# Another order of fills and loads at the head, a router table set in order once, and weight tiles copied two ahead

## The reference

```python
# 1. a recurrence over 768 steps, for 4 batches x 8 heads, head size 40
for t in range(S):
    y[:, :, t] = einsum('bhd,bhde->bhe', r_t, state)
    Sa    = einsum('bhde,bhe->bhd', state, a_t)
    state = state * w_t[:, :, None, :] - einsum('bhd,bhe->bhde', Sa, b_t) + einsum('bhd,bhe->bhde', v_t, k_t)
x = y as 3072 tokens of 320
# 2. first layer of experts: 8 experts, 320 -> 1024 -> 320
e_idx  = argmax(x @ w_gate);  gate = softmax(x @ w_gate)[e_idx];  eom = sigmoid(x @ w_output_gate)[e_idx]
out[token] = gate * eom * (relu(x[token] @ w1[e_idx]) @ w2[e_idx])
# 3. second layer, other weights, router w_gate2, with a capacity per expert (tokens past it give 0)
e_idx  = argmax(out @ w_gate2);  gate = softmax(out @ w_gate2)[e_idx]
out2[token] = gate * (relu(out[token] @ w1b[e_idx]) @ w2b[e_idx])
```

## Time and profile before

| | |
|---|---|
| median of 3 runs | 1327.27 us |
| the profiled execution | 1329.89 us, of which the span of the profile is 1328.1 us |
| busy in the span | PE 1088.1 us (82%), PEld 923.8, DVE 630.0 (47%), ACT 403.6 (30%), POOL 397.4 (30%) |
| granted TensorE clock, mean | 0.907 of full speed |
| chain that ended last | PE 51%, DVE 20%, DMA 11%, POOL 7%, issue 5%, ACT 3% |
| its largest lines | PE L1198 17%, PE L1179 10%, DMA of the first layer's gathers 8%, DVE L1477 6%, POOL L581 4%, DVE L1481 3% |
| L1477, 31 times | 149.4 us, 4820 ns each |
| L1481, 31 times | 87.4 us, 2820 ns each |
| stages by the timeline | head and first sets to 84 us, recurrence to 549 us, routing to 570 us, first layer to 974 us, routing to 1002 us, second layer to the end |

### The profile page before, as it was taken

How to read it: one execution, slowest core, us unless ns; L and a number is a source line. 1 busy time by engine, 2 the same in 40 slices (tenths; PEclk the granted TensorE clock), 3 DMA queues, 4 the chain that set the end, 5 groups by cost and what they waited for, 6 DMA issues and landing times.

```text
span 1328.1 us, 38352 instructions
## 1 busy us (share of the span) xinstructions
PE 1088.1 (82%) x16812; PEld 923.8 (70%) x16812; DVE 630.0 (47%) x864; ACT 403.6 (30%) x550; POOL 397.4 (30%) x278
## 2 busy tenths in 40 slices
PE   1288878787898899788688787879838999996997
PEld 0277778687788788577577676667617888875885
DVE  7546356654556451527657766757772111110111
ACT  0134333343433443133223222222103333323330
POOL 5543344423544300013332422432221121211111
PEclk9579889998988998889889988989968999998999
DMA  3433324434434221601233033212021322443000
GB/s 79 101 88 99 95 72 107 105 86 98 105 78 112 74 68 41 219 17 39 85 104 100 22 104 96 80 56 90 10 83 30 109 67 78 147 151 109 20 11 1
DMA packets 140870, 107.44 MB, mean 81 GB/s; under 512 B 89320, under 2 KB 118000, under 8 KB 140580
## 3 DMA queue, kind: packets, MB, share of 16 engines
q1 hardware_dynamic: 130560, 84.99, 23.6%
q0 software_dynamic: 6016, 16.05, 3.8%
q10 hardware_dynamic: 4132, 3.96, 1.0%
HBM read 87.51 MB, written 22.09 MB: 83 GB/s over the span
## 4 chain that ended last, share of the span: by engine, by line
PE 51%; DVE 20%; DMA 11%; POOL 7%; issue 5%; ACT 3%; SPq 1%; ACTq 0%; POOLq 0%; DVEq 0%
PE pair L1198 17%; PE pair L1179 10%; DMA y_T<-x_dram,token_all 8%; DVE AG L1477 6%; POOL AG L581 4%; DVE S_nat L1481 3%; DVE products L1265 3%; DVE T_rows L1270 3%; PE pair L1005 3%; PE pair L1186 3%; POOL abk_own L588 2%; PE pair L1166 2%; PE pair L926 2%; PE pair L1092 2%; PE pair L943 2%
## 5 line engine op out<-in xcount | busy, mean ns | idle before, releaser
L1198 PE MATMUL pair<-abk_own,H_nat 128*128 x992 | 302.6, 462 | 3.0 <-DVE S_nat L1470 1.7
L1198 PEld LDWEIGHTS pair<-abk_own,H_nat 128*128 128x128 f32 x992 | 197.2, 204 | 87.5 <-issue 25.0
L1179 PEld LDWEIGHTS pair<-H_nat,rvm 128*128 128x128 f32 x1984 | 239.8, 198 | 24.6 <-ACT H_nat L682 15.8
L1179 PE MATMUL pair<-H_nat,rvm 128*128 128x128 f32 x1984 | 241.2, 282 | 13.5 <-ACT H_nat L682 13.5
L682 ACT ACTIVATE rvm<-ring_own 128x2560 f32 x62 | 145.0, 2339 | 132.8 <-issue 80.6
L1477 DVE TENSOR_TENSOR AG<-AG,S_nat 128x2560 f32<-128x2560 f32 x31 | 149.4, 4820 | 1.1
L1470 DVE TENSOR_SCALAR S_nat<-pair,gate_all 128x320 f32<-128x320 f32 x62 | 34.2, 551 | 237.7 <-PE pair L1198 237.7
L833 ACT ACTIVATE H_nat<-pair 128x512 f32<-128x512 f32 x62 | 37.0, 597 | 329.0 <-PE pair L1186 329.0
L1463 DVE TENSOR_SCALAR H_nat<-pair 128x512 f32<-128x512 f32 x62 | 42.6, 687 | 170.3 <-PE pair L1186 170.3
L663 POOL DMA_INDIRECT between<-S_nat,token_all x31 | 35.8, 1155 | 267.1 <-DVE S_nat L1481 259.0
L581 POOL TENSOR_TENSOR AG<-abk_own,F_run 40x512 f32<-40x512 f32 x48 | 62.5, 1302 | 168.6 <-DVE T_nat L1273 152.9
(11 more groups left out here) (139 smaller groups left out, 1546.9 us busy)
## 6 DMA issues: line engine op xcount, KB each, us to landing
abk_own<-w SPq DMA_DIRECT2D x16, 1280.0 KB, 9.0
ring_own<-w SPq DMA_DIRECT2D x16, 512.0 KB, 3.5
ring_own<-w SPq DMA_DIRECT2D x32, 256.0 KB, 4.5
t_dram<-T_rows SPq DMA_DIRECT2D x12, 384.0 KB, 2.5
ring_own<-w SPq DMA_DIRECT2D x32, 128.0 KB, 5.2
w_in<-wT SPq DMA_DIRECT2D x48, 80.0 KB
abk_own<-aT SPq DMA_DIRECT2D x24, 160.0 KB
abk_own<-bT SPq DMA_DIRECT2D x24, 160.0 KB
```

The lines of the kernel that those rows point to most:

```text
L1179: mm(to, w1_now[:, par, k * F + m * P:k * F + m * P + P], xT[:, (0, 2 - m // 4)[k], :], start=(m % 4 == 0 and k == 0), stop=False, skip_gr ...
L1198: last = mm(bank[5][:, 0:DM], hidT[par][:, k, :], ring2[:, bass.ds(place, 1), k, :].rearrange("p a d -> p (a d)"), start=(k == 0), stop=(k ...
```

## The change

CLEARS falls from 6 to 4 and two fills get semaphores of their own (`abk_cleared`, `ag_cleared`): SP loads the first `a`, `b`, `k` when abk_own is clear, POOL starts when AG is clear. DVE fills AG first, makes the decays of set 0, and fills rvm, ZV and T_rows behind them (`clear_rest`). POOL's wait for the solve is left out for set 0. WARM is 9. The second router's weights are loaded to `wr_rows` as [320][8], and ACT copies them once to `wr_next` as [8][320]; L1477's product then reads both inputs with neighbouring elements. DVE waits for that copy before its first `relu1` of the first layer. `stage_w1` of the tile loop works on tile i+2 instead of i+3, in both layers; of the three copies ahead of the loop the third is dropped, and in the first layer the router copy stands in its place.

```diff
--- before.py
+++ after.py
@@ -65,7 +65,7 @@
 TABLES_IN = 16 * 2
 STEP_EXP, STEP_ONEHOT, STEP_SIG = 2, 6, 8
 AHEAD = 3
-WARM = 11
+WARM = 9
 BLK = 16
 NBLK = C // BLK
 SOLVE_STEPS = 2 * (BLK - 1) + 1
@@ -242,7 +242,8 @@
         ring2 = part(abk_own, 0, 2, FC, DM)
         A_flat = AG[:, :, :, :, :, :].rearrange("p u o b a t -> p (u o b a t)")
         terms = part(A_flat, 0, E, DM)
-        wr_next = part(A_flat, E * DM, DM, E)
+        wr_next = part(A_flat, E * DM, E, DM)
+        wr_rows = part(A_flat, 0, DM, E)
         w1_now = part(rvm[:, :, :, :, :].rearrange("p n b a t -> p (n b a t)"), 0, 2, W1_COLS)
 
         onehot, scratch, expo = (part(G_flat, n * NG * E, NG, E) for n in range(3))
@@ -269,6 +270,8 @@
 
         tables_in = sem("tables_in")
         cleared = sem("cleared")
+        abk_cleared = sem("abk_cleared")
+        ag_cleared = sem("ag_cleared")
         w_cleared = sem("w_cleared")
         ones_set = sem("ones_set")
         w_landed_in = sem("w_landed_in")
@@ -336,6 +339,7 @@
         lg_landed = sem("lg_landed")
         w_landed = sem("w_landed")
         wr_landed = sem("wr_landed")
+        wr_set = sem("wr_set")
         wr_turned = sem("wr_turned")
         router_in = sem("router_in")
 
@@ -389,7 +393,7 @@
         def fruns(k):
             return F_run[:, k % 4, :].rearrange("p (n t) -> p n t", t=C + 1)
 
-        CLEARS = 6
+        CLEARS = 4
         SLOTS = range(-3, NK + 1)
 
 
@@ -492,8 +496,10 @@
                         sp.wait_ge(f_scanned, load_set)
                     load_w(load_set)
                     if load_set == 0:
+                        sp.wait_ge(abk_cleared, 1)
+                if solves:
+                    if solve_set == 0:
                         sp.wait_ge(cleared, CLEARS)
-                if solves:
                     for u in (2 * solve_set, 2 * solve_set + 1):
                         if u >= 4:
                             sp.wait_ge(st_ready, states_upto(u - 4))
@@ -542,7 +548,7 @@
             sp.wait_ge(y_ready, NU)
             load_expert(0, 1)
             sp.wait_ge(wr_turned, 16)
-            sp.dma_start(wr_next, wr_dram.unsqueeze(0).to_broadcast([P, DM, E])).then_inc(wr_landed, 16)
+            sp.dma_start(wr_rows, wr_dram.unsqueeze(0).to_broadcast([P, DM, E])).then_inc(wr_landed, 16)
 
             for q in range(2, 2 * E):
                 s, e = divmod(q, E)
@@ -565,11 +571,12 @@
 
         @block.gpsimd
         def _(pool):
-            for t in (abk_own, T_T, S_nat):
+            nc.gpsimd.memset(abk_own[:, :], 0.0).then_inc(abk_cleared, 1)
+            for t in (T_T, S_nat):
                 nc.gpsimd.memset(t[:, :], 0.0).then_inc(cleared, 1)
             nc.gpsimd.memset(Z_diag, 0.0).then_inc(z_cleared, 1)
             nc.gpsimd.memset(D_nat[:, :], 0.0).then_inc(d_cleared, 1)
-            pool.wait_ge(cleared, CLEARS)
+            pool.wait_ge(ag_cleared, 1)
 
             def heads(t):
                 return t.rearrange("p b a t -> p (b a) t")
@@ -616,7 +623,7 @@
                 if grams:
                     pool.wait_ge(f_scanned, gram_set + 1)
                     pool.wait_ge(a_landed, 32 * (gram_set + 1))
-                    if nats:
+                    if nats and nat_set:
                         pool.wait_ge(solve_step, SOLVE_STEPS * (nat_set + 1))
                     for u in (2 * gram_set, 2 * gram_set + 1):
                         if u >= 5:
@@ -848,14 +855,15 @@
                 stage_w1(1, 1)
                 relu0(0, 0)
                 x_turned(1)
-                stage_w1(2, 0)
+                if s == 0:
+                    act.wait_ge(wr_landed, 16)
+                    copy(wr_next, wr_rows.rearrange("p d e -> p e d"), wr_set)
                 for i in range(MT):
                     if i + 1 < MT:
                         relu0(i + 1, (i + 1) % 2)
                     if i + 2 < MT:
                         x_turned(i + 2)
-                    if i + 3 < MT:
-                        stage_w1(i + 3, (i + 3) % 2)
+                        stage_w1(i + 2, i % 2)
 
 
         @block.tensor
@@ -1224,15 +1232,18 @@
             v.memset(w_in[:, ::C + 1], 0.0).then_inc(w_cleared, 1)
             dve.wait_ge(ones_set, 1)
             v.memset(ones_at[:, ::C + 1], 1.0).then_inc(ones_set, 1)
-            for t in (rvm, ZV, AG):
-                v.memset(t[:, :], 0.0).then_inc(cleared, 1)
-            v.memset(T_rows[:, :, :, :], 0.0).then_inc(rows_set, 1)
-            dve.wait_ge(tables_in, TABLES_IN)
-            dve.wait_ge(rows_set, 1)
-            v.tensor_copy(T_rows[:, :, :, BLK:2 * BLK], solve_init.unsqueeze(1).to_broadcast([P, 2, BLK, BLK])
-                          ).then_inc(rows_set, 1)
-            dve.wait_ge(cleared, CLEARS)
+            v.memset(AG[:, :], 0.0).then_inc(ag_cleared, 1)
             dve.wait_ge(ones_set, 3)
+
+            def clear_rest():
+                for t in (rvm, ZV):
+                    v.memset(t[:, :], 0.0).then_inc(cleared, 1)
+                v.memset(T_rows[:, :, :, :], 0.0).then_inc(rows_set, 1)
+                dve.wait_ge(tables_in, TABLES_IN)
+                dve.wait_ge(rows_set, 1)
+                v.tensor_copy(T_rows[:, :, :, BLK:2 * BLK], solve_init.unsqueeze(1).to_broadcast([P, 2, BLK, BLK])
+                              ).then_inc(rows_set, 1)
+                dve.wait_ge(cleared, CLEARS)
 
             def decays(k):
                 dve.wait_ge(w_landed_in, 64 * (k + 1))
@@ -1337,6 +1348,8 @@
                     m_out(2 * j)
                 if loads:
                     decays(j + 3)
+                if j == SLOTS[0]:
+                    clear_rest()
                 if chain:
                     y_out(2 * j)
                 if 0 < j <= NK:
@@ -1474,14 +1487,14 @@
                     dve.wait_ge(L["o_copied"][s], i + 1)
                     if i:
                         dve.wait_ge(lg_made, i)
-                    v.tensor_tensor(terms, wr_next.rearrange("p d e -> p e d"),
+                    v.tensor_tensor(terms, wr_next,
                                     y_rows[i % 2][:, 0:DM].unsqueeze(1).to_broadcast([P, E, DM]), ALU.mult
                                     ).then_inc(terms_made, 1)
                     dve.wait_ge(terms_made, i + 1)
                     v.tensor_reduce(y_rows[i % 2][:, DM:ROW], terms, AX_X, ALU.add).then_inc(lg_made, 1)
 
                 if s == 0:
-                    dve.wait_ge(wr_landed, 16)
+                    dve.wait_ge(wr_set, 1)
                 relu1(0, 0)
                 for i in range(MT):
                     if i + 1 < MT:
```

## The result

The changed kernel took 1225.56 us (median of 4 runs, 1220.02 to 1239.97); the kernel before, over its 4 runs, 1331.68 us. The profiled execution took 1228.57 us, its span 1226.8 us.

What follows compares the result with a forecast made beforehand. The first layer was taken as bound by a loop through DVE, POOL and DMA, not PE. From 1329.9 us profiled, -90 - 1.6 - 1.5 - 8.5 = -101.6 gave 1228 us; range 1216 to 1266.

Steps and rivals of the forecast that it cites:

- The product: DVE's L1477 in the first layer, reading neighbouring elements, falls from 4.82 us to 2.85.
- What follows from it: First layer: gather moves ahead of the next product, PE stops waiting, tiles come every 9.45 us; -93 us, net -90.
- The debit of 3 us: First layer: gathers beside experts' weight loads land later than the slack allows, 0.4 us for each of 7 loads.
- The first rival: First layer: gather stays behind the product, 14 pairs gain only 34 to 56 us, total 1262 to 1284; 28 in 100.
- The other two: Rivals: product gets no faster, 1318 us, 5 in 100; staging delays each tile's first `up`, up to 1355, 3 in 100.
- The page on POOL: Cited rule: POOL's SBUF interfaces are shared with DVE and contended by DVE instructions with two SBUF inputs, as the product remains.
- Staging two ahead: w1 copies in both layers: 0 generally, 0.8 us saved twice at second-layer experts of two tiles, -1.6 us.
- The router copy: ACT's copy ahead of the first layer's loop: 2.34 to 4.3 us long, covered before `down(0)`, cost 0.
- WARM 9: Fewer warming matmuls ahead of the routings: -1.5 us ahead of the first layer, 0 ahead of the second.
- The head: Kernel start, up to the first join: earlier first grams and POOL's wait left out, together -8.5 us.
- its two terms, -3.2 and -5.6: Head: first grams at 29.0 instead of 32.22, -3.2 us; first join no longer waiting for set 1's work, -5.6.
- my least value of 4.5: Head: smallest gain allowed for leaving out POOL's wait, since POOL now runs beside the first solve; 5.6 us was expected.

Runs made afterwards that it cites:

- the delays: Changed kernel with POOL filling a scratch buffer between the logits and each first-layer send: once, 1232.93 us; three times, 1282.23 us.
- the order alone: Kernel before, product still slow, with gather(i+4) issued ahead of send(i) instead of behind it: 1235.19 us, ratio 0.9307.

## Why the prediction was right, and where it was off

**The product** is right: 2.825 us against 2.85 taken. **What follows from it** is right, and it is the step that carried the result: D every 9.45, gathers at D - 1.0, `send` with the last one starting 311.0 us after the first gather, 92.5 less than before. Had only the product's length counted, 2 us in each of 31 tiles, the gain would have been some 60 us at most. The flip from behind to ahead of the next product is shown by the delays (3.5 us lost when the gather came 0.55 us later but still first, 53.5 when it came 2.6 later and behind the product's start) and by the order alone (89.7 us of the first layer without a faster product). The debit of 3 us for gathers beside weight loads did not fall due in the changed kernel: no later gather kept PE waiting.

**The first rival** (the gather stays behind the product) named the right mechanism and sized it from 34 to 56 us of gain; built on purpose, it left 403.5 - 364.5 = 39 us of gain in the first layer. The other two fell: the product did get faster, and no `up` of tiles 2 to 28 of the first layer waits for the copy.

**The page on POOL** (GPSIMD Engine Reference of the Trainium skill, the table of its section on specifications) was right to warn: the product with neighbouring reads, still one with two SBUF inputs, holds POOL, 3.41 instead of 1.0 where they meet.

**Staging two ahead** is right in kind. The copy ends 0.6 ahead of the end of `down`. At the experts of two tiles the next `up` starts when the copy ends:

```profile
1087.61 2.44 SPq L483 DMA_DIRECT2D ring_own<-w  x5
...
1098.77 2.34 ACT L689 ACTIVATE rvm<-ring_own 128x2560 f32 x1 [5.50 <-DMA abk_own<-w]
...
1101.21 5.18 PE L1187 MATMUL pair<-H_nat,rvm 128*128 128x128 f32 x32 [4.18 <-issue]
```

Before, a relu and an x copy stood between the earlier trace rows. The mean second layer over ten profiles with the new staging is 323.2 us, over four with the old 325.2: -2.0 against -1.6. Single profiles scatter by 2 us either way, since the `up` behind the wait ran at anything from 5.2 to 6.6 us.

**The router copy** is off in size and right in effect. ACT took

```profile
L689 ACT ACTIVATE rvm<-ring_own 128x2560 f32 x62 | 145.0, 2339 | 105.2 <-issue 85.5 <-DMA abk_own<-w 10.8 <-DMA ring_own<-w 8.9
...
L689 ACT ACTIVATE AG<-AG 128x2560 f32<-128x2560 f32 x1 | 4.9, 4860 | 0.0
```

4.86 us, 0.56 above my upper bound: ACT pays 0.98 ns for each element read 8 apart, where DVE paid 0.76. DVE's first relu waited for it until 579.14, 0.2 ahead of the end of the second `up`, and the first `down` started about 0.5 us later behind that `up` than before. So the cover was all but long enough, for a price that I had bounded from a DVE row.

**WARM 9** is the step that was wrong. I had costed it as work removed from the path, -1.5 and 0. Measured in this execution it is +1.3 and +3.9: 6.7 us off. What the step left out is what those matmuls are for. With 9 of them PE stood idle 0.8 and 2.2 us ahead of the lists' matmuls, and these then ran mostly at the lower of the two levels (1.2 instead of 2.4 GHz), 8.1 and 9.5 us, where the earlier trace rows were followed by 5.3. The first routing's lists in two stretches, with PE's busy time and behind it the granted clock:

```profile
551.83:554.50 2.67, 2.67 (x24) 1.00 0.00 0
554.50:559.91 5.41, 5.39 (x26) 0.50 0.00 0
```

The idle time is not the same in every execution. In the first routing the lists' matmuls are ready 9.8 us after the first warming matmul, in all six profiles with WARM 9. The nine warming matmuls take 8.8 to 10.0 us, the longer the later the higher clock is granted to them. So PE stood idle 0.8 to 2.4 us ahead of the eight lists that took 8.1 us or more, and not at all, 0.1, 0.7 and 1.1 ahead of the four that took 5.4 to 5.6. With WARM 11 it was at most 0.7, and all fourteen lists took 5.3 to 5.6. Idle times of 0.8 to 1.1 thus came before both. The two short lists of the profile with POOL's wait put back, after idle times of 0.1 and 1.1:

```profile
559.50 5.58 PE bank L1163 x48
...
898.10 5.58 PE bank L1163 x48
```

**The head** is right in sum (-8.4 in the mean of the profiles, -7.9 here, against -8.5; its two terms, -3.2 and -5.6, make -8.8) and was wrong in its split. After:

```profile
5.46 4.33 DVE L1235 MEMSET AG<- 128x5120 f32 x1 [1.00 <-issue]
...
10.57 2.33 DVE L1253 TENSOR_TENSOR_SCAN E_run<-w_in,ones_at 128x1041 f32<-128x1041 f32 x1 [0.79 <-DMA w_in<-wT]
...
15.70 4.93 POOL L588 TENSOR_TENSOR AG<-abk_own,F_run 40x512 f32<-40x512 f32 x4 [3.54 <-DVE F_run L1262]
...
29.03 1.16 PE L881 MATMUL pair<-abk_own,AG 64*64 64x64 f32 x64
...
37.56 4.42 POOL L595 TENSOR_TENSOR abk_own<-abk_own,E_run 128x1024 f32<-128x1024 f32 x2
...
39.95 2.04 DVE L1276 TENSOR_TENSOR products<-T_rows,G_rows 128x4 f32<-128x4 f32 x1
...
59.19 3.62 PE L934 MATMUL pair<-T_T,G_b 64*64 64x32 f32 x64 [15.76 <-DMA T_T<-t_dram]
```

AG is filled first, the E scan starts at 10.57 (10.3 taken), POOL at 15.70 (15.4), and the first grams at 29.03, as forecast. But the wait left out is worth 3.2, below my least value of 4.5, for a reason in these rows: POOL's scaling of set 1 (L595, 37.56 to 41.97) now runs beside the first solve, and one step of the solve took 2.04 us for its 4 elements instead of 0.17. The solve takes 11.3 us instead of 8.7. The rest of the head gave 5.1, above the 3.2 taken: the first grams come 4.0 earlier in the mean of the profiles (3.2 in this one), and another 1.0 was won behind them, where the grams ran at the higher clock (1.16 us against 1.99 in the earlier trace rows).

So the total met the forecast by 0.6 us on the profiled execution, but with errors that cancel: +6.7 for WARM, +0.6 for the head, -2.5 for the first layer, -2.4 for the second, -3.2 for a recurrence that happened to be shorter, and +1.0 on the way to the second routing. That it came so close is luck. One slip stands in the working: the 17 tiles of the earlier trace rows take 160.64 us, not 160.68, which changes nothing.

## What to carry to other kernels

Where a queue issues the next load behind a store that waits for the same tile's last result, look first at which instruction the load stands behind and what else will be running when it is issued. Compute from the rows how far each queued instruction is from the next collision: that margin (here 1.6 us from the gather's start to the product's) says whether an edit is worth its own length or, as 2 us a tile here were, a stall of 90 us over the layer. Don't count matmuls whose result nobody reads as waste until the trace shows that what runs behind them keeps its clock without them.

## What the runs showed of the hardware

A gather or scatter of 1.0 us that POOL starts while DVE multiplies two SBUF tensors ends 0.81 to 0.90 us after the product, whatever the product's length (4.83: 5.3; 2.83: 2.8 and 3.4). So it was in all 120 cases of the fourteen profiles. What started ahead of the product, by 0.1 to 1.0 us in 121 cases, was not held: the `send` at 647.11 above took 1.03 us, though the product began 0.4 us after it. It goes the other way too: the solve's product of 4 elements, started at 39.95 while POOL scaled `b` and `k`, ended at 41.99, with POOL's instruction (41.97).

A wait of PE can cost more than its length: 1.71 us of waiting was followed by a `down` 1.8 us longer (granted clock 0.73), as was the 3.60 of the earlier trace rows by one 1.3 longer (0.79).

The recurrence is the same code in all fourteen profiles from the first join on, and took from 474.7 to 493.5 us. That scatter, seen in the recurrence alone, is larger than the head's, the staging's and WARM's shares together; these were settled by their places in the traces, not by the medians. What makes it differ was not tried.
